# Folding rows s and S-s into sum and difference ahead of a two-step Fourier transform

## What is computed

```python
x = causal_conv7(x, softmax(weight))              # S = 4224 rows, D = 192 channels, 8 heads
u = x + (U @ V).T-mix of x over the sequence      # rank 32
x = u + relu(u @ w1a) @ w2a                       # first MLP, 192 -> 768 -> 192
X = np.fft.fft(x, axis=1)                         # over the 4224 rows
X = np.fft.fft(X, axis=2)                         # over the 192 channels
u = x + np.real(X)
un = (u - mean(u)) / sqrt(var(u) + 1e-6)
out = u + relu(un @ w1b) @ w2b                    # second MLP
```

## Time and profile before

| | |
|---|---|
| median of three timed runs | 1304.29 us (1303.7, 1304.29, 1307.62) |
| the profiled execution | 1301.41 us, of it span 1299.5 us |
| TensorE (PE) busy | 1270.2 us, 98% of the span, 9064 matmuls |
| VectorE (DVE) busy | 779.1 us, 60% |
| ScalarE (ACT) busy | 670.8 us, 52% |
| GpSimd (POOL) busy | 382.7 us, 29% |
| mean granted TensorE clock | 0.995 |

### The profile page before, as it was taken

How to read it: one execution, slowest core, us unless ns; L and a number is a source line. 1 busy time by engine, 2 the same in 40 slices (tenths; PEclk the granted TensorE clock), 3 DMA queues, 4 the chain that set the end, 5 groups by cost and what they waited for, 6 DMA issues and landing times.

```text
span 1299.5 us, 24641 instructions
## 1 busy us (share of the span) xinstructions
PE 1270.2 (98%) x9064; PEld 1251.3 (96%) x9064; DVE 779.1 (60%) x2045; ACT 670.8 (52%) x1594; POOL 382.7 (29%) x496
## 2 busy tenths in 40 slices
PE   6799999999999999999999999999999999999998
PEld 5799999999999999999999999999999999999998
DVE  5455565666655566555556666655566666665554
ACT  5355555444565555445555555544445555555553
POOL 0132321222233344322222244321102344443331
PEclk9899999999999999999999999999999999999999
DMA  9876542333457532224444222212233222232220
GB/s 300 258 263 204 167 146 90 122 124 116 151 191 245 168 104 67 63 81 134 125 121 130 85 86 92 78 60 86 87 99 102 83 84 88 84 94 83 69 78 29
DMA packets 89216, 157.21 MB, mean 121 GB/s; under 512 B 11192, under 2 KB 44096, under 8 KB 89052
## 3 DMA queue, kind: packets, MB, share of 16 engines
q1 hardware_dynamic: 85064, 149.22, 36.1%
q0 software_dynamic: 4032, 6.41, 1.6%
HBM read 96.68 MB, written 64.47 MB: 124 GB/s over the span
## 4 chain that ended last, share of the span: by engine, by line
PE 94%; DMA 2%; DVE 1%; SPq 1%; issue 1%; ACT 0%; POOLq 0%; POOL 0%; DVEq 0%
PE bank L698 19%; PE bank L699 9%; PE bank L679 8%; PE bank L687 7%; PE bank L686 7%; PE bank L683 7%; PE bank L680 7%; PE bank L732 4%; PE bank L702 4%; PE bank L780 3%; PE bank L701 2%; PE bank L750 2%; PE bank L749 2%; PE bank L748 2%; PE bank L764 2%; PE bank L817 1%
## 5 line engine op out<-in xcount | busy, mean ns | idle before, releaser
L1062 DVE SCALAR_TENSOR_TENSOR ht<-bank,ht 128x384 fp32r<-128x384 f32 x528 | 294.1, 557 | 378.6 <-ACT ht L880 374.6
L880 ACT ACTIVATE ht<-bank 128x384 fp32r<-128x384 f32 x528 | 259.8, 492 | 493.5 <-PE bank L687 492.9
L698 PE MATMUL bank<-w,ht 128*128 128x384 f32 x1320 | 418.3, 366 | 0.2
L699 PE MATMUL bank<-w,ht 128*128 128x192 f32 x1320 | 330.8, 251 | 0.0
L1274 POOL TENSOR_TENSOR ub<-ub,tmp 128x576 f32<-128x576 f32 x88 | 126.1, 1433 | 454.0 <-DVE ub L1070 302.3
L699 PEld LDWEIGHTS bank<-w,ht 128*128 128x128 f32 x1320 | 251.9, 191 | 0.0
L698 PEld LDWEIGHTS bank<-w,ht 128*128 128x128 f32 x1320 | 248.3, 188 | 2.8 <-issue 0.5
L679 PE MATMUL bank<-uth,w1h 128*128 128x384 f32 x528 | 189.1, 358 | 0.5 <-DVE w L1203 0.4
L687 PE MATMUL bank<-uts,w1t 128*128 128x384 f32 x528 | 179.7, 340 | 0.0
L686 PE MATMUL bank<-uts,w1s 128*128 128x384 f32 x528 | 178.9, 339 | 0.1
L683 PE MATMUL bank<-utl,w1h 128*128 128x384 f32 x528 | 178.6, 338 | 0.0
(11 more groups left out here) (112 smaller groups left out, 2396.6 us busy)
## 6 DMA issues: line engine op xcount, KB each, us to landing
f1t<-f_copy SPq DMA_DIRECT2D x44, 396.0 KB, 3.2
ub<-x_conv SPq DMA_DIRECT2D x44, 288.0 KB, 3.4
x_two<-ub SPq DMA_DIRECT2D x44, 288.0 KB
ub<-x_two SPq DMA_DIRECT2D x44, 288.0 KB, 3.1
mix<-mixed SPq DMA_DIRECT2D x44, 288.0 KB, 3.4
out<-ub SPq DMA_DIRECT2D x44, 288.0 KB
xin<-in_x SPq DMA_DIRECT2D x12, 864.0 KB, 6.6
x_conv<-xin SPq DMA_DIRECT2D x12, 756.0 KB
```

Source lines behind the costliest of these rows:

```text
L698: e.matmul(dn[t][:, 0:2 * D], hh, w2[ph][:, m, :], start=(m == 0), stop=False)
L699: mm = e.matmul(dn[t][:, 0:D], hl, w2[ph][:, m, 0:D], start=False, stop=False)
L880: e.activation(hth[q % 4], up[q % 3][:, 0:TOK], ACT.Relu).then_inc(act_h, 1)
L1062: e.scalar_tensor_tensor(htl[q % 4], up[q % 3][:, 0:TOK], 0.0, hth[q % 4].bitcast(F32), ALU.max, ALU.subtract).then_inc(dve_l, 1)
```

## The change

The cosine of a row's angle is the same for s and S-s, the sine has the other sign. The change adds and subtracts such rows ahead of the transform.

- Phase 0 blocks take other rows. Block 2k of a batch holds rows 33p + j for j = 3k+1 to 3k+3 ("rising"), block 2k+1 the rows S minus those ("falling"); block 10 holds j = 0, j = 16 and its mirror. Falling rows run against the partitions, so they are fetched and stored by indirect DMAs from POOL with row numbers from a table `back`: 24 fetches and 24 stores (five whole blocks and one tile a batch). SP loses those 20 loads and 20 stores.
- `fold` on DVE, once a pair of blocks, writes sum and difference (`xf`), 128 x 576 each, 20 times in all; the odd block has a short form of three operations on 128 x 192. The folded units, numbered w, take the place of blocks in `x2_high`, `x2_low`, `dft128` and `spectrum_*`. There are 11 a batch as before, with as many matmuls. Unit 9 is made in (0,b,10) slot 5 and transformed in the next block's slot 0, unit 10 made in that block's slot 1 and transformed in slot 4.
- `group_in` has three matmuls for each n (L896 to L898 of the new file): the low table part goes to columns of its own, next to the main result, and one of the three is 98 columns wide. `group_low` becomes a subtraction and an addition on 99 x 196 with a wait on `dve_tl` between them. `group_out` has three matmuls instead of six.
- `PUT_OFF` goes from 8 to 7; the tables `low`, `high`, `bc` halve; `u_free` also waits for the fold (`dve_xf`).

```diff
-PUT_OFF = 8
+PUT_OFF = 7
...
+def first_row(i, t):
+    if i == NB - 1:
+        return ((0, N2), (HALF, N2), (S - HALF, -N2))[t]
+    k = i // 2 * TB
+    return (k + 1 + t, N2) if i % 2 == 0 else (S - k - TB + t, -N2)
...
-        dft_at = {(n + 1, 4): n for n in range(LAST) if phase(n) == 0 and n not in later}
...
+                made = {NB - 2: (n0 + NB - 1, 5), NB - 1: (n0 + NB, 1)}.get(u, (n0 + u + 2, 1))
+                made_at[made] = w
...
+                    dft_at[{NB - 2: (n0 + NB, 0), NB - 1: (n0 + NB, 4)}.get(u, (n0 + u + 2, 4))] = w
...
         def u_free(e, n):
-            wait(e, u_out[n % UR], n // UR * 16)
+            if n >= UR:
+                landed(e, n - UR, u_out, fall_out)
+                if phase(n - UR) == 0:
+                    e.wait_ge(dve_xf, folded(n - UR))
...
-                    e.matmul(dst, flat[0][:, c], table(lowt, 0), start=True, stop=False, skip_group_check=True)
-                    e.matmul(dst, flat[0][:, c], table(lowt, 1), start=False, stop=False, skip_group_check=True)
-                    e.matmul(dst, flat[1][:, c], table(lowt, 0), start=False, stop=False, skip_group_check=True)
-                    e.matmul(dst, flat[2][:, c], table(hight, 0), start=False, stop=False, skip_group_check=True)
-                    mm = e.matmul(dst, flat[2][:, c], table(hight, 1), start=False, stop=True, skip_group_check=True)
+                    e.matmul(wide, flat[0][:, c], lowt[:, n], start=True, stop=False, skip_group_check=True)
+                    e.matmul(main, flat[1][:, c], lowt[:, n, 0], start=False, stop=False, skip_group_check=True)
+                    mm = e.matmul(wide, flat[2][:, c], hight[:, n], start=False, stop=True, skip_group_check=True)
...
-                for n in range(2):
-                    sh, sl = bct[:, 0, n, s:s + GR], bct[:, 1, n, s:s + GR]
-                    mh, ml = th[g % 2][:, n * 2 * CF:(n + 1) * 2 * CF], tl[g % 2][:, n * 2 * CF:(n + 1) * 2 * CF]
-                    e.matmul(o, sh, mh, start=(n == 0), stop=False)
-                    e.matmul(o, sl, mh, start=False, stop=False)
-                    mm = e.matmul(o, sh, ml, start=False, stop=(n == 1))
+                sh, sl = bct[:, 0, s:s + GR], bct[:, 1, s:s + GR]
+                e.matmul(o, sh, th[g % 2], start=True, stop=False)
+                e.matmul(o, sl, th[g % 2], start=False, stop=False)
+                mm = e.matmul(o, sh, tl[g % 2], start=False, stop=True)
...
+            def fold(n):
...
+                e.wait_ge(pool_y, n + 1)
+                wait(e, act_x2h, w - 1)
+                wait(e, dve_x2l, w - 1)
...
+                    x, y = u_slot(n - 1), u_slot(n)[:, ::-1, :]
+                    e.tensor_tensor(xf[:, 0], x, y, ALU.add).then_inc(dve_xf, 1)
+                    e.tensor_tensor(xf[:, 1], x, y, ALU.subtract).then_inc(dve_xf, 1)
...
-                e.tensor_tensor(tl[g % 2], o[0:GR, 0:4 * CF], th[g % 2].bitcast(F32), ALU.subtract).then_inc(tb_free[q], 1)
+                e.tensor_tensor(tl[g % 2], o[0:GR, 0:2 * CF], th[g % 2].bitcast(F32), ALU.subtract).then_inc(dve_tl, 1)
+                e.wait_ge(dve_tl, b * NG + g + 1)
+                e.tensor_tensor(tl[g % 2], o[0:GR, 2 * CF:4 * CF], tl[g % 2].bitcast(F32), ALU.add).then_inc(tb_free[q], 1)
...
+                    if m == 3 and n + 2 <= LAST and (backward(n + 2) or mixed_order(n + 2)):
+                        load_falling(n + 2)
```

More of the change, by code:

```diff
@@ L46 @@
 U_PARTS = [(0, PW), (PW, NT)]
-PUT_OFF = 8
+HALF = N2 // 2
+PUT_OFF = 7
 ROWS = 3
@@ L911, in spectrum_high @@
                     o, q = full(e, ("dft", n, half))
-                    copy(z[0:m, :, i * TB:(i + 1) * TB], o[0:m, 0:TB * 2 * KC].rearrange("p (t k) -> p k t", t=TB))\
-                        .then_inc(act_tb[q], 1)
+                    for rows, part in zip(spectrum_rows(z[0:m], n), spectrum_parts(o[0:m], n)):
+                        last = copy(rows, part)
+                    last.then_inc(act_tb[q], 1)
             def deviation(n):
@@ L1037, in _ @@
                         convolved_high(*piece)
-                    if m == 1 and pv is not None and phase(pv) == 0:
-                        x2_high(pv)
+                    if (n, m) in made_at:
+                        x2_high(made_at[(n, m)])
                     if m == 2 and nx is not None:
@@ L1250, in _ @@
                             group_rows(b, g)
-                    if m == 1 and pv is not None and phase(pv) == 0:
-                        x2_low(pv)
+                    if m == 1 and pv is not None and (backward(pv) or mixed_order(pv)):
+                        fold(pv)
+                    if (n, m) in made_at:
+                        x2_low(made_at[(n, m)])
                     if m == 1 and ahead(n, 2) is not None:
@@ L1297, in convolved_low, with falling, load_falling, store_falling @@
                 e.tensor_tensor(low, xin[p % 2][:, 0:w, cols], high.bitcast(F32), ALU.subtract).then_inc(pool_xl, 1)
+            def falling(n, t):
+                b, i = blocks[n][1:]
+                if mixed_order(n):
+                    return t[b], back[:, i // 2:i // 2 + 1], u_slot(n)[:, 2, :]
+                return (t[b].rearrange("(r t) d -> r (t d)", t=TB), back[:, i // 2:i // 2 + 1],
+                        u_slot(n).rearrange("p t d -> p (t d)"))
+            def load_falling(n):
+                u_free(e, n)
+                if blocks[n][2] == 1:
+                    x_stored(e, blocks[n][1])
+                rows, number, slot = falling(n, xc)
+                e.indirect_dma_start(slot, None, rows, bass.IndirectOffsetOnAxis(ap=number, axis=0)).then_inc(fall_in[n % UR], 16)
+            def store_falling(n):
+                e.wait_ge(pool_y, n + 1)
+                rows, number, slot = falling(n, x2d)
+                e.indirect_dma_start(rows, bass.IndirectOffsetOnAxis(ap=number, axis=0), slot, None).then_inc(fall_out[n % UR], 16)
             def mirror_rows(b, g):
@@ L1321, in v_low @@
                 a, z = (v * 128 for v in V_PARTS[n])
+                if n == 1:
+                    landed(e, 1, u_in, fall_in)
+                else:
+                    e.wait_ge(pool_y, 1)
                 e.wait_ge(v_h, n + 1)
```

216 lines of the change are left out of this document (143 added, 73 removed).

## The result

| | before | after the change |
|---|---|---|
| median of the timed runs | 1305.33 us (1303.7 to 1307.62) | 1271.58 us (1267.47 to 1273.8, 4 runs) |
| ratio, 95% interval | | 0.9737 [0.9705, 0.9768] |
| profiled execution, its span | 1301.41, 1299.5 us | 1272.86, 1271.0 us |
| mean granted TensorE clock | 0.995 | 0.987 |

The forecast was 1254 us, with a range of 1244 to 1270. The direction was right; the time lies 1.6 us outside the range. (Before was timed again beside it, hence its 1305.33 us.)

A forecast was written before the change was run, and what follows sets the result against it. TensorE was taken as the bound, its own instructions making 94% of the chain. 1301.4 - 56.2 (matmuls) + 3.3 (unit 9) + 2.5 (block 3's fetch) = 1251.0 us, 1254 for the median; range 1244 to 1270.

The forecast's parts named there:

- The matmuls removed: 352 fewer matmuls in `group_in` at 91.0 ns and 264 fewer in `group_out` at 91.7 ns: 56.2 us gained.
- The narrow matmul at 0: 176 matmuls of 98 instead of 196 columns gain 0, since loading weights sets the pace; upper end of gain 8.4 us.
- The rival of 1246 us: Columns streamed set the narrow matmul's price, so 8.4 us more are gained; chance 0.12.
- "I take 0", for the fold on DVE: The fold's 1.52 us a pair, 30.4 us in all, hides in DVE's 29.5 us idle ahead of `x2_low`: cost 0.
- `group_low` and `INSIDE`, 0, ends 0 and 3: `group_low`'s second operation, 11 us on DVE, costs 0; where batch 1's groups meet folds, 0 to 3 us in all.
- DVE becomes the bound in places: Rival: DVE gets 46 us more work; if half shows, 1271 us; chance 0.15.
- Block 1's fetch goes out as soon as its rows are stored, as before from SP: Block 1's fetch, now issued by POOL, goes out as before; no cost was added for it.
- The fetch of block 3, 2.5, ends 1.1 and 4.2: Block 3's fetch stands behind `vlate` on POOL, so TensorE stands still once near 75 us: 2.5 us, between 1.1 and 4.2.
- Unit 9, 3.3 with 0 at the first transition: Unit 9, squeezed between two slots, costs 1.1 us at three of four transitions: 3.3 us, ends 0 and 10.4.
- The gathers hidden in the steady state: POOL's fetches for block n+2 have 11.2 us before `make_u` wants them: cost 0, hidden by 6 us.
- The rival of 1325 us: Gather time grows with bytes to 14.4 us, `make_u` is 3.2 us late 24 times, 77 us slower; chance 0.03.
- `u_free`'s wait for the fold, 0: It holds SP about a slot at some second-phase loads, which are issued three blocks ahead: cost 0.

The follow-up runs named there:

- e4_wide: Changed kernel with the narrow 98-column matmul of a group given its 196 columns back: 1273.62 us, ratio 0.9764.
- e1: Changed kernel with POOL adding a block's mixed rows (`add_mixed`) in slot 4 of the block before, so not beside the fold's sum: 1264.68 us, ratio 0.9688.
- e5: Changed kernel with unit 10 made a slot later and unit 9 transformed in slot 1 instead of slot 0, every batch: 1273.86 us, ratio 0.9763.
- e6: Changed kernel with `group_low` as one operation, the low table part computed but not added: 1269.26 us, ratio 0.9721.
- e3: Changed kernel with POOL's first gather (block 1) held back until the weights `w2` have landed: 1272.31 us, ratio 0.9762.
- e8: Changed kernel with the first phase's second weights loaded three transfers earlier on SP, ahead of the wait for the stored v part: 1270.35 us, ratio 0.9727.
- e2: Changed kernel with block 3 fetched right after the first `add_partial`, and `vlate` waiting for that fetch: 1266.18 us, ratio 0.9694.
- e12_split: Changed kernel with only the fold's difference moved to slot 2 behind `turned_low`: 1274.91 us, ratio 0.9769.
- e9_three: Changed kernel with the edits of e1, e2 and e8 together: 1255.42 us, ratio 0.9614.
- e10_four: e9_three plus, in batch 0 alone, unit 9's transform in slot 1 of block 11 instead of slot 0: 1251.86 us, ratio 0.9593.

## Why the prediction was wrong, step by step

- **The matmuls removed**: right, 91 ns each, and 1.93 us a block where nothing is in the way. The total of 56.2 us stands.
- **The narrow matmul at 0**: right, by e4_wide and by the starts. The rival of 1246 us is out. Of the two sections of the Trainium skill that I had weighed ("TensorE: Matmul & The Clock Gate"), the trace agrees with the one on the stationary operand's load: 91 ns for 98 and for 196 columns alike, near its 82.5 ns for 99 loaded columns.
- **"I take 0", for the fold on DVE**: this step failed. The cover held where it was read, ahead of `x2_low`: the 29.5 us of wait fell to 16.6, and blocks of batches 2 and 3 with a fold alone lost nothing. But the step asked only whether DVE had time, not with whom it shares what it reads through. Where `fold` met POOL's `add_mixed`, it was held for the whole of it. That is 4.5 and 3.3 us at two places (e1: 7 us), slow clock included, with no term in my sum. The Trainium skill says so ("SBUF — State Buffer", section "SBUF: two separate sides"): DVE and GpSimd share a port pair, and a DVE operation with two inputs in SBUF and a GpSimd operation lock each other out. The trace agrees on the lock, in both directions, with 2.25 us for 0.75 and 0.59 to 0.76 us for 0.2. By the page the operation that starts first gets the ports. The records here don't show that: the held sum begins 0.18 us ahead of `add_mixed`. Two operands are not the only case here: the copy of e5, with one, was held too. `add_mixed` stands in slot 0 of (0,b,10) on POOL and `fold` in slot 1 on DVE: looked up, it would have been a term.
- **`group_low` and `INSIDE`, 0, ends 0 and 3**: failed; it gave back 5.8 us. I compared averages over a block (1.9 us more on DVE against 1.9 less on TensorE and 5.6 idle). What decides in the blocks with a fold is one stretch, from `group_low` in slot 1 to `turned_low` in slot 2, in which DVE has no idle time at all. They give back 3.7 us, 1.1 a block and so just over my upper end, and e6 shows 1.65 of it to be `group_low`'s second operation; that the rest is the fold was argued and not shown. Blocks 14, 16 and 18, for which I had allowed nothing, give back 2.0 us in one of their two lengths and nothing in the other, and what decides between these stays open. My rival "DVE becomes the bound in places" had the right kind here, at a quarter of its 23 us. That it also gave 1271 us is chance.
- **"Block 1's fetch goes out as soon as its rows are stored, as before from SP"**: failed. SP had it 0.5 us behind `load_w2`, POOL issues it at the same moment, in queues that are full, and block 0 ends 5.2 us later. That the gather alone does this is not shown: delayed (e3) it gave back 1.3 us of the wait and nothing of the block. 3.4 us come back when the weights are moved (e8).
- **The fetch of block 3, 2.5, ends 1.1 and 4.2**: right mechanism and place, mis-sized: 7 us (e2). POOL was free only at 74.21 us, 3.0 later than in the rows that I had used, the landing was 6.7 us, just above my upper end, and behind a wait of 5.3 us came a clock of 0.67 over 10 us, for which I had no term.
- **Unit 9, 3.3 with 0 at the first transition**: without the collision 2.0, 0.0, 2.5 and 2.4 us, 6.9 in all, inside my ends of 0 to 10.4. The waits of TensorE on `x2l` that I had named as the sign don't show at any of them. So the total lies inside the ends, at twice the 3.3 that I took, without the mechanism being shown. The first transition, for which I took nothing, waited 1.7 us, and for a bank that `make_u` frees, not for `x2l`.
- **The gathers hidden in the steady state**: right. The 24 land in 4.1 us (median), and DVE's only long wait for one is block 3's. The rival of 1325 us is out.
- **`u_free`'s wait for the fold, 0**: right by a hair. e12_split shows what stands behind it: TensorE waited 0.27 us for that table in the changed kernel and 2.6 us with the fold's difference one slot later.

By size, the sum's excess of 21.9 us is 8.0 in the first blocks, 7.8 for the lock, 3.6 for the other part of the transitions, 5.8 for `INSIDE`, less 3.5 of drift that helped (21.7). Much of the first two is slow clock (3.4 us behind the sum of block 43 alone), which stood in none of my terms. With the lock and both early transfers mended, e9_three takes 1255.4 us, and e10_four 1251.9.

## To carry to other kernels

Where TensorE runs 98% busy, give a new wait a chance of a slow clock behind it: here one of 1.5 us cost 3.4 us more. Before costing an added DVE operation at nothing, look at what POOL does in the same stretch: here a sum of two SBUF operands and a copy of one were held for the whole of an addition on POOL. An operation newly issued on POOL, such as an indirect store, also moves what stands behind it. And ask for the longest stretch without a pause ahead of the operation that the bound engine waits for, not for idle time per block.

## What the hardware showed

- DVE and POOL held each other up, one operation at a time, by about the full length of the other's: on DVE a sum of two SBUF operands (0.75 us became 2.25 beside 1.44 us) and a copy of one (0.25 became 1.76 beside 1.44, e5_unit9), on POOL operations of 0.2 us (0.59 to 0.76).
- A standstill of TensorE of 1.5 us was followed by 8 us mostly at the 1.2 GHz level. Whether it is, varies: the same wait of 1.7 us in block 11 was followed by a clock of 1.00 in the changed kernel, and by 0.50 over 5 us in e2_fetch3_early. A wait of 1.6 us in block 32, there before the change too, was followed by 1.00 in most kernels and by 0.83 over 10 us in e4, e5, e8 and e9, with the block 1.5 us longer. So one trace of a kernel can be a few us off its others at such places. The changed kernel's runs spread over 6.3 us, and those of e10_four over 1.5. That the waits make the spread is not shown: e1, which keeps those of blocks 2 and 11, spreads over 1.3.
- Behind a 98-column matmul the next starts after about 45 ns and the one after it about 135 ns later; behind 196 columns each takes 90. What sets the 91 ns on average was not measured by itself: the number of loaded columns was not changed.
